# Normalization moved to ScalarE, low parts of the output weights to GpSimd, and a new order around the last chunk of a three-stage kernel

## The reference

```python
def _moe_ref(x, w_a, w_b, w_out):                  # d_ff = 1536
    return (x @ w_a) * (x @ w_b) @ w_out
def _moe2_ref(x, w_in, w_out, g_ln):               # d_ff = 1024
    h = x @ w_in
    e = np.exp(h - np.max(h, axis=-1, keepdims=True))
    solu = h * (e / (np.sum(e, axis=-1, keepdims=True) + 1e-09))
    mu = np.mean(solu, axis=-1, keepdims=True)
    var = np.mean((solu - mu) ** 2, axis=-1, keepdims=True)
    ln = (solu - mu) / np.sqrt(var + 1e-06) * g_ln
    return ln @ w_out
```

## Time and profile before

| what | us |
|---|---|
| median of 3 runs (lowest to highest) | 1003.35 (1000.21 to 1003.78) |
| the profiled execution | 1002.53 |
| its span in the trace | 1000.7 |
| PE busy in the span | 968.9 (97%) |
| DVE busy | 572.5 (57%) |
| ACT busy | 431.4 (43%) |
| POOL busy | 327.2 (33%) |
| share of PE in the chain that ended last | 90% |

### The profile page before, as it was taken

The page is one execution under the profiler, slowest core; times in us unless marked ns, Lnnn a source line. Parts: engine busy times, 40 slices in busy tenths (PEclk is TensorE's granted clock), DMA queues, the critical chain, the costliest instruction groups (busy, mean ns, idle before and its releaser), DMA issues.

```text
span 1000.7 us, 16650 instructions
## 1 busy us (share of the span) xinstructions
PE 968.9 (97%) x5790; PEld 920.5 (92%) x5790; DVE 572.5 (57%) x912; ACT 431.4 (43%) x761; POOL 327.2 (33%) x314
## 2 busy tenths in 40 slices
PE   5999999999999999999999999999998989999997
PEld 4999999999998999999999999999998768888876
DVE  6788788878778644222222222222235697888883
ACT  3777777777778543212112112112123433333331
POOL 2777777777778100000000000000002434433320
PEclk9999999999999999999999999999999889999999
DMA  6666666666762543110010010000020200000001
GB/s 177 159 160 163 157 157 157 158 162 161 168 136 56 168 127 95 32 33 1 0 31 0 0 31 0 0 0 0 1 84 7 78 22 22 21 21 21 21 22 42
DMA packets 51572, 71.40 MB, mean 71 GB/s; under 512 B 14552, under 2 KB 24920, under 8 KB 51536
## 3 DMA queue, kind: packets, MB, share of 16 engines
q1 hardware_dynamic: 51536, 70.94, 27.4%
HBM read 33.25 MB, written 5.32 MB: 39 GB/s over the span
## 4 chain that ended last, share of the span: by engine, by line
PE 90%; DVE 5%; issue 1%; DMA 1%; ACT 1%; SPq 1%; POOL 0%; DVEq 0%
PE PS L1291 12%; PE PS L1308 10%; PE PS L1309 10%; PE PS L1310 10%; PE PS L1253 9%; PE PS L1255 8%; PE PS L1375 5%; PE PS L1376 5%; PE PS L1377 5%; PE PS L1397 3%; PE PS L1399 3%; PE PS L1398 3%; PE PS L1449 3%; PE PS L1447 3%; PE PS L1448 3%; PE PS L1435 2%
## 5 line engine op out<-in xcount | busy, mean ns | idle before, releaser
L564 POOL TENSOR_TENSOR p_lo<-prob,p_hi 128x576 fp32r<-128x576 f32 x144 | 207.9, 1445 | 50.3 <-ACT p_hi L694 48.4
L1253 PE MATMUL PS<-ops 128*128 128x288 f32 x642 | 182.0, 305 | 15.0 <-DVE ops L1017 6.6
L1308 PE MATMUL PS<-x_hi,w_ab_rolled 128*128 128x384 f32 x576 | 192.5, 334 | 0.2 <-DVE w_ab_rolled L973 0.2
L1309 PE MATMUL PS<-x_lo,w_ab_rolled 128*128 128x384 f32 x576 | 192.4, 334 | 0.0
L1310 PE MATMUL PS<-x_hi,w_ab_rolled 128*128 128x384 f32 x576 | 192.4, 334 | 0.0
L1056 DVE TENSOR_TENSOR gate<-gate,PS 128x384 f32<-128x384 f32 x72 | 39.9, 554 | 245.6 <-ACT gate L798 245.6
L1255 PE MATMUL PS<-ops 128*128 128x288 f32 x642 | 177.2, 297 | 0.0
L798 ACT ACTIVATE gate<-PS 128x384 f32<-128x384 f32 x72 | 35.4, 492 | 264.8 <-PE PS L1310 264.8
L609 POOL TENSOR_TENSOR y_sums<-xT 128x256 f32<-128x256 f32 x9 | 6.6, 737 | 429.6 <-PE PS L1310 429.5
L1253 PEld LDWEIGHTS PS<-ops 128*128 128x128 f32 x642 | 122.2, 190 | 24.3 <-issue 12.2
L941 DVE TENSOR_REDUCE neg_max<-PS 128x1 f32<-128x576 f32 x144 | 108.4, 755 | 59.9 <-PE PS L1255 59.7
(11 more groups left out here) (114 smaller groups left out, 1661.5 us busy)
## 6 DMA issues: line engine op xcount, KB each, us to landing
qk_raw<-qkT_dram SPq DMA_DIRECT2D x32, 288.0 KB, 3.0
ops<-qk_hi SPq DMA_DIRECT2D x62, 144.0 KB
ops<-qk_hi SPq DMA_DIRECT2D x31, 288.0 KB
ops<-qk_lo SPq DMA_DIRECT2D x62, 144.0 KB
v_raw<-v_tiles_dram SPq DMA_DIRECT2D x32, 160.0 KB, 2.7
xT<-head_sb SPq DMA_DIRECT2D x32, 144.0 KB, 3.2
out_dram<-o_sb SPq DMA_DIRECT2D x18, 256.0 KB, 2.0
stage<-inverse_dram SPq DMA_DIRECT2D x20, 192.0 KB, 3.7
```

The lines of the kernel that those rows point to most:

```text
L564: pool.tensor_tensor(p_lo[:, s, :], prob[:, s, :], p_hi[:, r, :].bitcast(F32), ALU.subtract).then_inc(p_lo_done, 1)
L1253: pe.matmul(ps[:, b, 0:HALF], weights[0][:, r, own], moving[0][:, r, cols], start=(n == 0), stop=False)
L1308: pe.matmul(bank, w[:, 0, :], x_hi[:, k, :], start=(k == 0), stop=False)
L1309: pe.matmul(bank, w[:, 0, :], x_lo[:, k, :], start=False, stop=False)
```

## The change

Normalization becomes one ACT instruction, Identity with a scale (the factor) and a bias (minus mean times factor, a new one-column DVE instruction). `solu` gets two places. The scale by `g_ln` is applied in place on `w_out` by ACT in the last chunk (`scale_wout`), the high part is a plain copy after it, and the low part is a subtraction on POOL instead of DVE. The first two loads move forward. The high and low parts of y for pair 0 are made from block 9 of the last chunk on; blocks 10 and 11 of that chunk have places of their own for the gate product (`g_last`), and `hidden(0)` stands before all three last `down`s. At the end each turn stands between two halves of a project. The buffers are laid out anew.

```diff
-        stage = sb(outer, "stage", [P, 3, FK])
+        with ExitStack() as same:
+            stage = sb(same, "stage", [P, 3, FK])
+        g_last = sb(outer, "g_last", [P, 2, 2, CH], F32R)
...
+            with ExitStack() as same:
+                wout_raw = sb(same, "wout_raw", [P, NK2, DM])
+            solu_1 = sb(a, "solu_1", [P, F2])
...
+            expo_0 = sb(a, "expo_0", [P, F2])
             expo_1 = sb(a, "expo_1", [P, F2])
-            expo_0 = sb(a, "expo_0", [P, F2])
-            solu = sb(a, "solu", [P, F2])
+            solu_0 = sb(a, "solu_0", [P, F2])
             normed = sb(a, "normed", [P, F2])
...
+        def g_part(parts, n, c, f):
+            return g_last[:, f % 2, n, :] if c is LAST_CHUNK and f >= NF - 2 else parts[:, f % 2, :]
...
-            sp.wait_ge(ab_done, (NCH - 1) * NF + W_IN_FREE)
+            sp.wait_ge(ab_done, LAST + 2)
             sp.dma_start(win_raw[:, :, :], w_in.rearrange("(k p) n -> p k n", p=P)).then_inc(win_in, 16)
-            sp.wait_ge(win_lo, 7)
+            sp.wait_ge(y_done, LAST + 4)
             sp.dma_start(wout_raw[:, :, :], w_out.rearrange("(k p) n -> p k n", p=P)).then_inc(wout_in, 16)
...
+            def low_wout(ks):
+                for k in ks:
+                    pool.wait_ge(wout_hi, k + 1)
+                    pool.tensor_tensor(wout_lo_sb[:, k, :], wout_raw[:, k, :], wout_hi_sb[:, k, :].bitcast(F32),
+                                       ALU.subtract).then_inc(wout_lo, 1)
...
+            pool.wait_ge(y_done, LAST + 8)
+            pool.memset(halfpow[:, :], -0.5).then_inc(half_set, 1)
             low_y(0)
-            pool.memset(halfpow[:, :], -0.5).then_inc(half_set, 1)
+            sum_y(1)
+            pool.wait_ge(win_lo, 7)
+            low_wout(range(5))
+            low_y(1, (0, 1))
             pool.wait_ge(half_set, 1)
-            sum_y(1)
-            low_y(1, (0, 1))
             rstd(0, 0)
             low_y(1, (2, 3))
+            low_wout(range(5, 7))
             rstd(0, 1)
+            low_wout(range(7, NK2))
```

ACT and DVE:

```diff
-                at_least(act, y_done, NF * c + f - 1)
-                act.activation(g_hi[:, f % 2, :], gate[:, :], ACT.Copy).then_inc(g_hi_done, 1)
+                if not (c is LAST_CHUNK and f >= NF - 2):
+                    at_least(act, y_done, NF * c + f - 1)
+                act.activation(g_part(g_hi, 0, c, f), gate[:, :], ACT.Copy).then_inc(g_hi_done, 1)
...
+            def scale_wout(ks):
+                for k in ks:
+                    act.wait_ge(wout_in, 16)
+                    act.activation(wout_raw[:, k, :], wout_raw[:, k, :], ACT.Copy, scale=gain[:, k:k + 1]).then_inc(wout_scaled, 1)
...
-                    act.activation(wout_hi_sb[:, k, :], wout_raw[:, k, :], ACT.Copy, scale=gain[:, k:k + 1]).then_inc(wout_hi, 1)
+                    act.wait_ge(wout_scaled, k + 1)
+                    act.activation(wout_hi_sb[:, k, :], wout_raw[:, k, :], ACT.Copy).then_inc(wout_hi, 1)
...
+            def normed_step(p, j):
+                n = 2 * p + j
+                act.wait_ge(norm_ready, n + 1)
+                at_least(act, turned, n)
+                act.activation(normed[:, :], solu[j][:, :], ACT.Identity, bias=small[:, 6:7], scale=small[:, 5:6]).then_inc(normed_done, 1)
...
                 out_copy(p - 1, 0)
+                normed_step(p, 0)
                 if final:
                     high_normed(p, 0)
                 out_copy(p - 1, 1)
                 if not final:
                     high_normed(p, 0)
...
+                normed_step(p, 1)
+            high_x(NCH - 1)
+            y_out(NCH - 2)
+            for f in range(NF):
+                high_gate(LAST_CHUNK, f)
+                for b in {6: (B11, B21), 7: (B22,), 8: (T3,), 9: (T2,), 11: (T4,)}.get(f, ()):
+                    high_win(b)
+                scale_wout({7: range(3), 8: range(3, 6), 9: range(6, NK2)}.get(f, ()))
+                if f == 9:
+                    act.wait_ge(y_done, LAST + 8)
+                    act.wait_ge(y_out_dve, (NK // 2) * 2)
+                    high_y(0, (0,))
+                if f == 10:
+                    high_y(0, (1, 2))
+                    high_win(T1)
             copy_first(0)
+            high_wout()
+            act.wait_ge(y_done, LAST + 9)
             expo_step(0, 0)
             high_y(1, (0,))
+            act.wait_ge(y_done, LAST + 10)
             expo_step(0, 1)
             high_y(1, (1, 2))
             y_out(NCH - 1, range(NK))
+            normed_step(0, 0)
             copy_first(1)
+            act.wait_ge(g_lo_done, NF * NCH)
             high_normed(0, 0)
-            high_wout()
+            normed_step(0, 1)
             high_normed(0, 1)
...
+                at_least(dve, normed_done, n)
                 link(n, 5, dve.tensor_scalar(small[:, 5:6], small[:, 3:4], small[:, 1:2], None, ALU.mult))
-            def normed_step(p, j):
-                n = 2 * p + j
-                at_least(dve, turned, n)
-                dve.tensor_scalar(normed[:, :], solu[:, :], mean_var[:, 0:1], small[:, 5:6],
-                                  ALU.subtract, ALU.mult).then_inc(normed_done, 1)
+                dve.tensor_scalar(small[:, 6:7], mean_var[:, 0:1], small[:, 5:6], -1.0, ALU.mult, ALU.mult).then_inc(norm_ready, 1)
...
                 hidden_sums(p)
+                if isinstance(p, int) and p == 0:
+                    dve.wait_ge(y_done, LAST + 11)
                 solu_step(p, 0)
                 norm_step(p, 0)
-                normed_step(p, 0)
-                dve.wait_ge(normed_done, 2 * p + 1)
+                if isinstance(p, int) and p == 0:
+                    dve.wait_ge(wout_lo, 2)
                 solu_step(p, 1)
...
+                elif final:
+                    stats_step(p, 1)
+                    low_normed(p, 0)
+                    small_steps(p, 1)
...
             low_normed(0, 0)
             late_sums(1)
-            low_wout(range(NK2))
             low_normed(0, 1)
```

PE:

```diff
                 pe.wait_ge(ya_lo_done, 4 * p + 1)
                 at_least(pe, solu_done, 2 * p - 1)
+                if first:
+                    pe.wait_ge(g_done, NF * NCH - 1)
                 product_of(p, A11, B11, 1, first)
                 product_of(p, A12, B21, 0, first)
...
-            chunk(NCH - 1, last=True)
-            down(NCH - 1, NF - 3)
-            pe.wait_ge(g_done, NF * NCH)
-            hidden(0, first=True)
-            down(NCH - 1, NF - 2)
-            down(NCH - 1, NF - 1)
+            chunk(LAST_CHUNK, last=True)
+            hidden(0, {}, first=True)
+            for f in range(NF - 3, NF):
+                down(LAST_CHUNK, f)
             pe.wait_ge(consts_in, 48)
-            hidden(1, ((0, 0), (0, 1)))
+            hidden(1, {2: (0, 0), 7: (0, 1)})
...
+            hidden(last, {4: (last - 1, 1)})
+            first_half, second_half = range(NK2 // 2), range(NK2 // 2, NK2)
             project(last - 1, 0)
+            project(last - 1, 1, ks=first_half)
             turn(last, 0)
-            project(last - 1, 1)
+            project(last - 1, 1, ks=second_half)
+            project(last, 0, ks=first_half)
             turn(last, 1)
-            project(last, 0)
+            project(last, 0, ks=second_half)
             project(last, 1)
```

More of the change, by code:

```diff
@@ L182, in build_program @@
                 win_raw = sb(same, "win_raw", [P, NK, F2])
-            wout_raw = sb(a, "wout_raw", [P, NK2, DM])
+            wout_lo_sb = sb(a, "wout_lo_sb", [P, NK2, DM], F32R)
             win_blocks = sb(a, "win_blocks", [P, 4, 2, 2, BANK], F32R)
         expo = (expo_0, expo_1)
+        solu = (solu_0, solu_1)
         B11, B21, B22, T3, T2, T1, T4 = range(7)
@@ L1237, in _ @@
                 pair_tiles(p)
-            pair_tiles(last)
-            low_normed(last, 0)
+            pair_tiles(last, final=True)
             low_normed(last, 1)
@@ L1374, in down @@
                     w = w_od[:, f, :, m * P:(m + 1) * P]
-                    pe.matmul(bank, w[:, 0, :], g_hi[:, f % 2, :], start=(f == 0), stop=False)
-                    pe.matmul(bank, w[:, 0, :], g_lo[:, f % 2, :], start=False, stop=False)
-                    ins = pe.matmul(bank, w[:, 1, :], g_hi[:, f % 2, :], start=False, stop=(f == NF - 1))
+                    high, low = g_part(g_hi, 0, c, f), g_part(g_lo, 1, c, f)
+                    pe.matmul(bank, w[:, 0, :], high, start=(f == 0), stop=False)
+                    pe.matmul(bank, w[:, 0, :], low, start=False, stop=False)
+                    ins = pe.matmul(bank, w[:, 1, :], high, start=False, stop=(f == NF - 1))
                 ins.then_inc(y_done, 1)
@@ L1400, in product_of, with hidden @@
                 ins.then_inc(h_part, 1)
-            def hidden(p, turns=(), first=False):
+            def hidden(p, turns, first=False):
                 pe.wait_ge(ya_lo_done, 4 * p + 1)
                 at_least(pe, solu_done, 2 * p - 1)
+                if first:
+                    pe.wait_ge(g_done, NF * NCH - 1)
```

(28 more changed lines are left out.)

75 lines of the change are left out of this document (30 added, 45 removed).

## The result

| | before | after |
|---|---|---|
| median, us (lowest to highest, runs) | 1003.0 (1000.21 to 1003.78, 4) | 987.61 (986.77 to 988.2, 4) |
| the profiled execution | 1002.53 | 988.2 |
| its span | 1000.7 | 986.4 |
| PE / DVE / ACT / POOL busy | 968.9 / 572.5 / 431.4 / 327.2 | 963.5 / 553.4 / 456.9 / 333.4 |
| granted clock, mean of the span | 0.991 | 1.00 |

After over before is 0.9851, 95% interval [0.983, 0.9872]: 15.4 us less; 988.5 was predicted.

The account below looks back on a forecast made before the run. PE was taken as the bound, busy 97% of the span, so only its waits and half-clock time could be won. 13.8 + 2.95 - 2.2 = 14.5 off 1002.5 gave 988.0, stated as 988.5; range 984 to 994.

Parts of the forecast that it names:

- the six us behind it: First turn, (0, 0): after `down(10)`, DVE starts `solu` at 783.4, normalization follows, and the turn starts at 789.45.
- The term of 13.8: Start of the last layer through the turn of (1, 0): after that turn 811.25 against an equivalent 825.05, 13.8 us saved.
- that of 2.95: End of the kernel, turns of (8, 0) and (8, 1): finish at 994.4 against 997.35, 2.95 us saved.
- T1's low part 1.22 ... to 770.2: DVE's work for `hidden(0)`: T1's low part takes 1.22 us and ends at 770.2.
- the first rival: First layer turns: GpSimd becomes the bound, its low parts taking 2.16 and the power 1.4 late: 993; chance 0.15.
- The clock's 2.2: Lower clock behind three remaining waits of 1.3 to 1.5 before turns: 2.2 us lost, the middle between the bounds.
- The early parts: Second rival, before `hidden(0)`: ACT's longer queue delays the last gate rows, so `hidden(0)` starts as before: 995 to 998; chance 0.09.
- the third rival: Loop: ACT's copy for the next pair, behind normalization, comes late; at worst 2.7 per pass, 19 in all: 1007; chance 0.04.
- The fourth: At all three waits before turns: the clock stays up and hops are short: 985 or just below; chance 0.10.

Follow-up runs that it names:

- The exchange of places: Changed kernel with the two `solu` buffers' places exchanged, so the weights of `down(10)` lie under `solu_1` and the second tile waits for them: 985.89 us.
- late parts of y: Changed kernel with high parts of y made after block 11, T1 and T4 in block 10, `down(9)` ahead of `hidden(0)`, last gate rows waiting again: 992.53 us.
- the first edit: Changed kernel with all three high parts of y for pair 0 in block 9 and POOL's `sum_y(1)` behind T4: 986.96 us.

## Why the prediction was right, and where it was not

Its steps, with distances from the gate copy of block 11 so that the start drops out:

| step | predicted | measured |
|---|---|---|
| start of `hidden(0)` | -0.2 | -0.20 |
| wait in it, between starts | 0.65 | 1.48 (1.32 in the view) |
| DVE may begin `solu` (after `down(10)`) | 14.41 | 15.51 |
| turn of (0, 0), its wait | 20.46, 1.3 | 21.59, 1.23 |
| from there to the turn of (1, 0), its wait | 20.90, 1.3 | 20.77, 1.03 |
| pass of the loop | 22.19 | 22.19 |
| end: turn of (7, 1) to last `o_sb` | -2.95 | -2.90 |
| waits at (8, 0), (8, 1) | 1.5, 0.5 | 1.42, 0.19 |
| normalization on ACT | 1.21 | 1.24 |
| low part of `w_out` on POOL | 1.30 | 1.26 |
| clock | -2.2 | 0 |

**The chain of waits held.** What ends each wait was named rightly: the second sum, `down(10)` and the six us behind it, the sum after the turn of (0, 1), the normalization at the end. The exchange of places shows the second of these; late parts of y show what the early start is worth. The term of 13.8 came out as 12.75, that of 2.95 as 2.90.

**The wait in `hidden(0)` was mis-sized, by 0.8.** The step was "T1's low part 1.22 ... to 770.2". It took 2.28 and ended 2.00 behind the gate copy where 1.21 was worked out; T4's low part took 1.39 for 1.2, and the second sum ended 0.9 late. The prediction weighed the two engines' meeting for POOL's work alone, and only at `w_out`. It had POOL's first two low parts of y end before 769.5, 0.5 behind the gate copy (the second ended 0.9 behind it, the third 2.6), and did not ask what they do to DVE. Holding POOL back removed what the first edit had left of this wait, so this cause is shown. Another 0.1 lies in the first four products, 5.57 us for 24 matmuls where 5.45 was taken. The view's 1.32 is smaller than the 1.48 between the starts because it counts from the end of the last record, 0.39 long, while a matmul costs 0.23.

**The small values.** ACT's normalization at 1.24, against bounds of 1.03 and 1.50, cost 0.03 more than the estimate. The row that leads to it is that of the exponential: one column operand added 0.09 to a copy out of PSUM (1.03). The normalization reads SBUF, and against a copy out of SBUF (1.045 in the same trace) two operands added 0.20. The Trainium skill ("ScalarE: Activation LUTs", "What ACT_TABLE_LOAD costs") gives about 93 ns for each such operand; the trace agrees, with 92 ns for one and 201 for two. POOL's low parts of `w_out` beside DVE's work out of PSUM took 1.26, no longer than the 1.30 of POOL alone, so the first rival did not come. It was nearer than worked out: POOL began these 7.45 behind the gate copy where the prediction has 4.7, because its four sums for pair 1 (773.64 to 777.75), which the prediction leaves out, stand ahead of them. POOL was free 1.06 before the input of the first power came.

**The clock's 2.2 was not paid.** The prediction took the middle between 0 and 4.4. In all eight executions of the changed kernel the mean clock was 0.998 or more, and in the two profiled ones no stretch is low. (Two others have 0.998. In other kernels here a mean of 0.998 without a fall behind a wait goes with 0.91 in the first 20 us; for these two no trace tells.) Waits behind which a lower clock is on record: 3.57, 1.65 (with 0.20 after it), 3.85, 3.46, then 4.12, 2.10, 3.52, 2.32 in the experiments. Waits behind which it stayed: 1.03 to 1.42 here, then 1.45, 1.72, 1.81, 2.10, 2.50, 2.69, 3.04. No wait under 1.65 was followed by a fall, and each of 3.46 or more was; between them length alone does not decide. What does is open. The middle between the bounds was a choice without a row, and the first rival's "surely falls for waits of over 2 us" does not hold either.

**The hit is part cancellation.** The distance fell by 15.65 where 16.75 was worked out (14.5 with the clock's 2.2 taken off). The sum missed 1.1, the clock gave back 2.2, and the gate copy came 1.27 later in this execution, which no step foresaw: the span fell by 14.3 beside a forecast of 14.5. A right time is not yet right terms.

**The other rivals.** The early parts came early: the last gate copy on ACT stood 0.31 for PE and for nothing in its own queue. The loop did not get slower, and one extra normalization of 1.24 per tile costs it 0.32 a pass, far from the 2.7 of the third rival at its worst. The fourth, clock up and short hops, is half what happened.

## What to carry to other kernels

Follow the chain of the late engine instruction by instruction and ask of each who else works out of the same memory then: a helper with slack can stretch the engine that has none, and holding it back a microsecond costs nothing as long as its own queue is not what is waited for next. Where two such instructions meet, look at which begins first: here that one lost little, and the other waited. Undo each part of a change, since the one that gives it its name (normalization on ScalarE, worth nothing) need not be the one that pays (the order at the two ends of the last layer). Where two edits fit each other, as the split projects and the place of ACT's last normalization behind an output copy, undo them together, or the mismatch is measured.
